# Retention, mixture of experts and a cosine layer on one core: the first unit's tiles joined by two engines, one transposed tile moved a slot

## The reference

```python
ret = scale * (q @ k.T) * Dmat            # gamma ** (i - j), lower triangle, 4 x 8 heads of 576 x 64
x = (ret @ v)                             # as 2304 rows of 512
noisy = x @ w_gate + log1p(exp(x @ w_noise)) * noise
top2 = two largest of the 8 experts; top2_w = softmax of the two
x = sum over the two: top2_w * (relu(x @ w1[e]) @ w2[e])      # 512 -> 1024 -> 512
h = x @ w_in                              # 512 -> 2048
out = (h * cos(h)) @ w_out                # 2048 -> 512
```

## Time and profile before

| what | value |
| --- | --- |
| median of 3 runs | 964.06 us (963.14 to 966.89) |
| profiled execution, its own time | 964.38 us |
| its span, first to last instruction | 962.5 us |
| TensorE busy | 936.7 us (97%) |
| VectorE, ScalarE busy | 560.2 us (58%), 534.7 us (56%) |
| mean granted TensorE clock | 0.987 |

### The profile page before, as it was taken

How to read it: one execution, slowest core, us unless ns; L and a number is a source line. 1 busy time by engine, 2 the same in 40 slices (tenths; PEclk the granted TensorE clock), 3 DMA queues, 4 the chain that set the end, 5 groups by cost and what they waited for, 6 DMA issues and landing times.

```text
span 962.5 us, 16768 instructions
## 1 busy us (share of the span) xinstructions
PE 936.7 (97%) x5984; PEld 834.6 (87%) x5984; DVE 560.2 (58%) x1118; ACT 534.7 (56%) x969; POOL 95.9 (10%) x93
## 2 busy tenths in 40 slices
PE   8999859999999999999999998999999999999998
PEld 8988858888888889898989888888988888888897
DVE  4788635465655555533331244567777777776665
ACT  2556537554655556453532256566757765766555
POOL 2276500000000000000000222001100100000000
PEclk9999879999999999999999999999999999999999
DMA  9999465779999999985427357877666755656561
GB/s 361 330 327 283 176 163 197 204 236 302 314 309 321 324 307 296 259 257 156 103 73 263 98 196 264 295 286 255 235 250 237 264 213 228 239 210 238 216 236 55
DMA packets 113113, 230.44 MB, mean 239 GB/s; under 512 B 47384, under 2 KB 71640, under 8 KB 104856
## 3 DMA queue, kind: packets, MB, share of 16 engines
q1 hardware_dynamic: 107288, 210.73, 65.6%
q0 software_dynamic: 5760, 18.88, 5.5%
HBM read 157.65 MB, written 61.70 MB: 228 GB/s over the span
## 4 chain that ended last, share of the span: by engine, by line
PE 76%; ACT 7%; DVE 7%; issue 4%; DMA 2%; POOL 1%; SPq 1%; DVEq 0%; POOLq 0%; ACTq 0%
PE ps L1708 17%; PE ps L1690 16%; PE ps L1877 13%; PE ps L1863 11%; PE ps L1791 3%; PE ps L1803 2%; PE ps L1614 2%; PE ps L1637 2%; ACT angle L984 2%; PE ps L1726 2%; PE ps L1629 2%; PE ps L1662 2%; DVE angle L1473 1%; ACT angle L982 1%; PE ps L1738 1%
## 5 line engine op out<-in xcount | busy, mean ns | idle before, releaser
L1877 PE MATMUL ps<-w_sb,g_hi 128*128 128x512 f32 x576 | 180.4, 394 | 0.1
L1690 PE MATMUL ps<-xs,w_hi 128*128 (+1 forms) x784 | 173.3, 303 | 0.8 <-DVE hs_lo L1297 0.8
L1690 PEld LDWEIGHTS ps<-xs,w_hi 128*128 128x128 f32 x784 | 131.2, 188 | 4.2 <-DVE hs_lo L1297 1.2
L1303 DVE TENSOR_TENSOR w_lo<-raw,w_hi 128x1024 fp32r<-128x1024 f32 x48 | 58.8, 1225 | 124.1 <-ACT w_hi L823 124.0
L1863 PE MATMUL ps<-x_odd,w_sb 128*128 128x320 f32 x672 | 117.7, 310 | 2.2 <-DVE h_sb L1458 1.2
L1863 PEld LDWEIGHTS ps<-x_odd,w_sb 128*128 128x128 f32 x672 | 106.2, 188 | 14.5 <-DVE h_sb L1458 2.5
L1690 PE MATMUL ps<-xs,w_lo 128*128 (+1 forms) x392 | 118.8, 303 | 0.0
L823 ACT ACTIVATE w_hi<-raw 128x1024 fp32r<-128x1024 f32 x48 | 50.9, 1060 | 118.0 <-PE ps L1708 113.1
L1877 PE MATMUL ps<-w_sb,g_lo 128*128 128x512 f32 x288 | 112.5, 391 | 0.0
L1877 PEld LDWEIGHTS ps<-w_sb,g_hi 128*128 128x128 f32 x576 | 101.0, 188 | 9.8 <-issue 0.3
L1708 PE MATMUL ps<-w_hi,hs_lo 128*128 128x512 f32 (+1 forms) x245 | 96.8, 395 | 0.0
(11 more groups left out here) (195 smaller groups left out, 1624.8 us busy)
## 6 DMA issues: line engine op xcount, KB each, us to landing
w_sb<-w_pairs SPq DMA_DIRECT2D x24, 1792.0 KB, 7.9
w_sb<-w_pairs SPq DMA_DIRECT2D x40, 1024.0 KB, 9.6
raw<-weights SPq DMA_DIRECT2D x64, 512.0 KB, 4.9
w_pairs<-stage SPq DMA_DIRECT2D x24, 1024.0 KB, 7.1
qk<-qk SPq DMA_DIRECT2D x18, 512.0 KB, 7.2
kv<-kv SPq DMA_DIRECT2D x18, 512.0 KB, 5.9
y_slots<-zeros_sb SPq DMA_DIRECT2D x33, 256.0 KB
raw_pair<-pairs SPq DMA_DIRECT2D x8, 1024.0 KB, 9.2
```

The costliest lines, as they stand in the source:

```text
L1303: tt(w_lo[:, at], raw[:, f % 2, :], w_hi[:, at].bitcast(F32), ALU.subtract).then_inc(split_done, 1)
L1690: last_one = nc.tensor.matmul(ps[5 + half][:, 0:HALF], w[:, at:at + P], xs[:, bass.ds(g % 2, 1), a, k, half * HALF:(half + 1) * HALF].rear ...
L1877: last_one = nc.tensor.matmul(ps[j][:, :], a[:, slot % 2, part, j * C:(j + 1) * C], w2_sb[slot % 3][:, hl, part * DM:(part + 1) * DM], sta ...
```

## The change

Unit 0's tiles are joined by two engines: ScalarE copies the lower plane (join in its stream), VectorE the upper (its own join, with a semaphore merged_dve). The tiles 2 to 4 get a buffer each, in raw_pair[1], in place of the one x_plain. On ScalarE the order in step 18 becomes: both joins, high part of tile 0, x_sb copy of tile 16, high part of tile 1. On VectorE the joins of tiles 0 and 1 stand ahead of second_choice and behind sum_picks. place_results goes behind the first h_low_first of part 1. From unit 1 on the joins stay on ScalarE. In block 0 of the last layer the third tile goes through one slot later on all engines.

```diff
--- before.py
+++ after.py
@@ -281,6 +281,7 @@
         passed, passed_sp = sem("passed"), sem("passed_sp")
         gath_in = [sem(f"gath_in{i}") for i in range(TPU)]
         merged, xs_hi_done, xs_done = sem("merged"), sem("xs_hi_done"), sem("xs_done")
+        merged_dve = sem("merged_dve")
         h_done, relu_done, hs_done = sem("h_done"), sem("relu_done"), sem("hs_done")
         p2_done, y_ready = sem("p2_done"), sem("y_ready")
         y_act, y_dve = sem("y_act"), sem("y_dve")
@@ -432,7 +433,19 @@
 
             if isinstance(g, int) and g == 0 and j < FRONT[0]:
                 return planes[FRONT[0] + j][:, :, :].rearrange("p a s -> p (a s)").bitcast(F32)
+            if isinstance(g, int) and g == 0:
+                return raw_pair[1][:, (j - FRONT[0]) * DM:(j - FRONT[0] + 1) * DM]
             return x_plain[:, :]
+
+        def half_of(g, j, h):
+
+            n = KD_TILES * ROWS[j]
+            return (x_raw(g, j)[:, 0:n].bitcast(U16).rearrange("p (k s h) -> p h k s", k=KD_TILES, h=2)[:, h, :, :],
+                    planes[j][:, h * KD_TILES:(h + 1) * KD_TILES, 0:ROWS[j]])
+
+        def joined(g, j):
+
+            return j + 1 if isinstance(g, int) and g == 0 else 2 * (TPU * g + j + 1) - TPU
 
         def steps_before(g):
 
@@ -562,14 +575,18 @@
             for j in range(FRONT[0], TPU):
                 load_rows(j, 0)
             for j in range(FRONT[0]):
-                sp.wait_ge(merged, 2 * (j + 1))
+                sp.wait_ge(merged, j + 1)
+                sp.wait_ge(merged_dve, j + 1)
                 load_rows(j, 1)
             for f in range(2):
                 load_chunk(RING + f, FE + f)
             for j in range(FRONT[0], TPU):
-                sp.wait_ge(merged, 2 * (j + 1))
+                sp.wait_ge(merged, j + 1)
+                sp.wait_ge(merged_dve, j + 1)
                 load_rows(j, 1)
             def load_pair(i):
+                if i == 1:
+                    sp.wait_ge(xs_done, TPU)
                 if i >= 2:
                     sp.wait_ge(pair_lo, 3 * (i - 1))
                 sp.dma_start(raw_pair[i % 2][:, :], pairs[i]).then_inc(pair_in[i % 2], 16)
@@ -592,14 +609,14 @@
                 e_next = nc.sync.value_load(meta[0:1, bass.ds(g + 1, 1)], min_val=0, max_val=E - 1)
                 v_next = nc.sync.value_load(meta[0:1, bass.ds(g + META_V + 1, 1)], min_val=0, max_val=NV - 1)
                 for j in range(2):
-                    sp.wait_ge(merged, 2 * (TPU * g + j + 1))
+                    sp.wait_ge(merged, joined(g, j))
                     sp.sem_inc(passed_sp, 1)
                     load_rows(j, v_next)
                 for j in range(TPU):
                     store_rows(g - 1, j)
                 for f in range(FE):
                     if 2 <= f < TPU:
-                        sp.wait_ge(merged, 2 * (TPU * g + f + 1))
+                        sp.wait_ge(merged, joined(g, f))
                         sp.sem_inc(passed_sp, 1)
                         load_rows(f, v_next)
                     load_ring(g, f, e_next)
@@ -768,19 +785,25 @@
                 if k < NG - 1:
                     nc.scalar.activation(sin_ready[:, :], tab("half_pi"), ACT.Exp)
 
+            def join(g, j):
+                act.wait_ge(gath_in[j], 16 * g + 16)
+                first = isinstance(g, int) and g == 0
+                if isinstance(g, int) and g == 1 and j == 0:
+                    act.wait_ge(y_pos_done, 1)
+                if not first:
+                    act.wait_ge(xs_done, TPU * g + j)
+                for h in range(1 if first else 2):
+                    to, half = half_of(g, j, h)
+                    nc.scalar.activation(to, half, ACT.Copy).then_inc(merged, 1)
+
             def x_high(g, j):
-                act.wait_ge(gath_in[j], 16 * g + 16)
-                if not isinstance(g, int) or g > 0 or j > FRONT[0]:
-                    act.wait_ge(xs_done, TPU * g + j)
-                n = KD_TILES * ROWS[j]
-                for h in range(2):
-                    nc.scalar.activation(
-                        x_raw(g, j)[:, 0:n].bitcast(U16).rearrange("p (k s h) -> p h k s", k=KD_TILES, h=2)[:, h, :, :],
-                        planes[j][:, h * KD_TILES:(h + 1) * KD_TILES, 0:ROWS[j]], ACT.Copy).then_inc(merged, 1)
-                act.wait_ge(merged, 2 * (TPU * g + j + 1))
+                act.wait_ge(merged, joined(g, j))
+                if isinstance(g, int) and g == 0:
+                    act.wait_ge(merged_dve, j + 1)
                 nc.scalar.activation(
                     xs[:, bass.ds(g % 2, 1), 0, :, rows_of(j)].rearrange("p a k s -> p (a k) s"),
-                    x_raw(g, j)[:, 0:n].rearrange("p (k s) -> p k s", k=KD_TILES), ACT.Copy).then_inc(xs_hi_done, 1)
+                    x_raw(g, j)[:, 0:KD_TILES * ROWS[j]].rearrange("p (k s) -> p k s", k=KD_TILES), ACT.Copy
+                    ).then_inc(xs_hi_done, 1)
 
             def step(s):
                 if s in SOFT_AT:
@@ -793,8 +816,9 @@
                     nc.scalar.activation(xT[t % 2][:, :, :], ps[O_BANK[t % 2]][:, :].rearrange("p (k c) -> p k c", k=KD_TILES),
                                          ACT.Copy).then_inc(xT_done, 1)
                 if t == NT - 1:
-                    for j in range(FRONT[0]):
-                        x_high(0, j)
+                    join(0, 0)
+                    join(0, 1)
+                    x_high(0, 0)
                 t = s - 2
                 if t == NT - 1:
                     softplus(NG - 1)
@@ -803,6 +827,8 @@
                     nc.scalar.activation(x_sb[t][:, :].bitcast(U16).rearrange("c (h d) -> c h d", h=2),
                                          ps[5][0:C, :].bitcast(U16).rearrange("c (d h) -> c h d", h=2), ACT.Copy
                                          ).then_inc(x_done, 1)
+                if t == NT - 2:
+                    x_high(0, 1)
                 if s in SPLIT_AT:
                     split_high(SPLIT_AT[s], w_hi, SPLIT_AT[s] * CHUNK)
 
@@ -853,12 +879,14 @@
                     act.wait_ge(g_ready, 1)
                     nc.scalar.activation(gate2[:, 0:NT], g_a[:, :], ACT.Exp).then_inc(g_done_exp, 1)
             for j in range(FRONT[0], TPU):
+                join(0, j)
                 x_high(0, j)
             for f in range(FE):
                 relu_first(f, 1)
                 if f > 0:
                     ring_high(f - 1)
                     if f <= TPU:
+                        join(1, f - 1)
                         x_high(1, f - 1)
             relu(FE, 0)
             y_rows(0)
@@ -886,6 +914,7 @@
                         y_rows(g)
                     w_high(g, f)
                     if f < TPU:
+                        join(g + 1, f)
                         x_high(g + 1, f)
                     if isinstance(g, int) and g <= PREP_UNITS:
                         pair_high(2 * (g - 1) + f // 4, f % 4)
@@ -1001,9 +1030,10 @@
                 first = FIRST_TILE[b + 1]
                 if b == 0:
                     if p == 2:
-                        for j in range(3):
+                        for j in range(2):
                             copy_raw(first + j)
                     if p == 3:
+                        copy_raw(first + 2)
                         prepare(first + 3)
                         prepare(first + 4)
                         x2_high(1, 0)
@@ -1044,6 +1074,7 @@
                 cosine(slot, 1)
                 if slot == 1:
                     prepare(FIRST_TILE[1] + 1)
+                if slot == 2:
                     prepare(FIRST_TILE[1] + 2)
             for slot in range(FP, SLOTS + 1):
                 b, p = slot // FP, slot % FP
@@ -1180,6 +1211,11 @@
                     nc.vector.tensor_tensor(ret[t % 3][rows, half, :, :], scores[rows, :, :],
                                             decay[rows, half, :, :], ALU.mult).then_inc(ret_done, 1)
 
+            def join(j):
+                dve.wait_ge(gath_in[j], 16)
+                to, half = half_of(0, j, 1)
+                nc.vector.tensor_copy(to, half).then_inc(merged_dve, 1)
+
             def carry(t):
                 c = t % CB
                 dve.wait_ge(u_done, updates(t) + 1)
@@ -1211,9 +1247,13 @@
                     carry(s - 1)
                 if s < NT and s % CB < CB - 1:
                     decay_k(s)
+                if s == NT:
+                    join(0)
                 if s in SECOND_AT:
                     second_choice(SECOND_AT[s])
                     sum_picks(SECOND_AT[s])
+                if s == NT:
+                    join(1)
                 if s in PLACE_AT:
                     place_rows(PLACE_AT[s])
                 if s in FIRST_AT:
@@ -1337,12 +1377,13 @@
                     list_units()
                 if f == 6:
                     gates()
-                if f == 7:
-                    place_results()
             for j in range(FRONT[0], TPU):
+                join(j)
                 x_low(0, j)
             for f in range(FE):
```

(8 more changed lines are left out.)

## The result

| | before | changed kernel |
| --- | --- | --- |
| median | 964.06 us (963.09 to 966.89, 5 runs) | 958.1 us (956.68 to 959.6, 5 runs) |
| ratio, 95% interval | | 0.9934 [0.9914, 0.9955] |
| profiled execution, its own time | 964.38 us | 958.10 us |
| its span | 962.5 us | 956.3 us |
| mean granted TensorE clock | 0.987 | 0.993 |

A forecast was written before the change was run, and what follows sets the result against it. TensorE bounds the kernel, working 936.7 of 962.5 us, so gains lie where it stands or runs at lower clock. 1.2 + 2.2 + 4.2 = 7.6 off 964.38 gives 956.8, median 956.5 us; range 953.5 to 960.8.

The forecast's parts named there:

- Front: Up to the experts' first product: joins shared by ScalarE and VectorE start it near 100.9 instead of 102.09, 1.2 us less.
- Late tiles: Unit 0's tiles 2 to 4: joins side by side in own buffers shorten the chain from 8.1 to 5.9, 2.2 us less.
- place_results and the clock: Part 1 and after restarts: moving place_results costs zero; both low-clock costs kept, a 3 us longer stretch costing 1.5 us.
- zero, nothing is moved past another transfer: SP's queue: waits come at the same points, met earlier, and load_pair(1) waits for late tiles long done; zero.
- a sign of being wrong: Unit 1: an unforeseen wait at the h_low behind place_results or at the ring loads would make the prediction wrong; no size.
- Block 0: Last layer, third tile one slot later: 2.7 us of standing and the lower clock behind it go, 4.2 us less.
- It waits for nothing: Slot 3 of block 0: third tile ready after 5.1 us, TensorE at its transposes after 6.3, 1.2 us to spare.
- the wait comes back: Block 0, slot 3 or 4: third tile's combine or the weights come late, 4.2 us falls away, 960.7; chance 0.11.
- The front's rival: VectorE's first copy, blocked by up to 0.96 us beside a scatter, delays second_choice; 0.2 of the term left, 957.5; chance 0.10.
- Slow copies with every other element: VectorE's five chain copies: from 2.2 us a copy the gain is gone, at 3.2 it ends at 969; chance 0.03.
- The late tiles don't land too slowly: Unit 0: late tiles land one by one and joins wait for them, the 2.2 falls to about zero, 958.7; chance 0.04.
- The clock's rival: Both restarts get the long low-clock stretch, or block 0's idle cost no clock in the typical run: 959; chance 0.08.

The follow-up runs named there:

- one_buffer: Changed kernel with both engines joining, but one x_plain for all late tiles and place_results back in its old place; 960.1 us, ratio 0.9946.
- place_back: Changed kernel with place_results back in its old place ahead of the late tiles; 958.75 us, ratio 0.9942.
- ring_first: Changed kernel with SP's first ring load of unit 1 issued ahead of the five stores of unit 0's rows; 957.49 us, ratio 0.992.
- prep_later: Changed kernel with scaling and combining of block 1's fifth tile in slot 3 placed behind x2_high and x2_low; 959.01 us, ratio 0.992.
- prep_turn: Changed kernel with block 1's fifth tile scaled behind the second half's turn of slot 3 and combined behind its reduce; 956.94 us, ratio 0.9912.
- tile: Kernel before with only block 0 changed, its third tile one slot later, unit 0 as before; 965.0 us, ratio 0.9981.
- unit0: Changed kernel with only the part on unit 0, block 0's third tile back in its old slots; 961.34 us, ratio 0.9949.

## Why the prediction came out as it did

The forecast was right in kind, and 1.6 us too far. That it came so near is in part luck: in the table above, the terms that turned out larger than forecast (front, late tiles, clock, block 0 up to slot 4) have 1.4 us in its favour, and those that it put at nothing 2.7 against it.

*Front (1.2 forecast, 1.66 measured).* The mechanism held: the low part of tile 1 sets the first product, behind ScalarE's row. The price of the VectorE copy, 0.45 in place of 0.68, isn't what the size was off by, since both copies are done before ScalarE's high parts want them. The sum added up whole durations on ScalarE: from the start of the joins to the end of the second high part 3.74 us (96.36 to 100.1). It measured 3.29 (96.64 to 99.93), because each instruction that waits for nothing begins some 0.1 us before the one ahead has ended. Those are the 0.45. The kernels with the new front all show 4.55 to 4.57 us from the last xT copy to the first product, also those in which TensorE waited 0.4 to 1.1 us for the x_sb copy. The exception is one_buffer with 5.18, where both engines begin their joins of tile 1 only at 99.39.

*Late tiles (2.2 forecast, 2.56 measured).* From the first join to the end of the last low part the sum had 5.9 us, and it measured 5.55. The two VectorE copies on this chain gave 0.17 of the difference, the low parts 0.23 and the high parts 0.06 (again each begins before the one ahead has ended), and ScalarE's first join took 0.11 more. The Trainium skill (VectorE: DVE Perf Modes, on the 2x mode with both ports) would have given 2.9 by its copy of 0.33 us. The measurement lies between: the copy takes 0.45 us for 512 elements and 0.39 for 416. I estimate from these two that 0.32 of the 0.45 goes with the length, and some 0.13 us is there whatever the length, near the smallest operations of the earlier trace rows (0.18). The same page remarks beside its table that the fixed part of a single operation was measured at about 150 cycles; from that I would have estimated 0.42, and the runs agree with it better. The three buffers or the second engine alone give some 70% of the gain (1.85 and 1.74 of 2.56), as the runs with one of the two show.

*place_results and the clock (0).* The first is confirmed by place_back. As for the clock, the stretch at 1.2 GHz behind the first product lasts to 104.5 (3.8 us, before 3.3) and the one behind the late tiles to 138.6 (5.4 us, before 6.2). The first costs under 0.1 us and the second gives 0.4, inside the 1.5 that I left open.

*SP, "zero, nothing is moved past another transfer".* **This step failed**, by 0.7 us in the profile and by 0.7 and 0.4 in the two repeats (in the other kernels that leave unit 1 alone, 0.02 to 1.04). Nothing was moved in SP's queue. The five stores begin at 172.25, 3.96 us earlier than before (176.21), as much as TensorE is ahead. But their issues take 3.70 us in place of 3.16, and from the load behind them to ScalarE's split of its weights it is 5.0 us in place of 4.8, so the split comes only 3.17 us earlier. ring_first shows that this queue bounds unit 1, as it did before the change. Why the stores and the load take longer now stays open. The prediction named a wait in unit 1 at the ring loads as a sign of being wrong, and didn't price it.

*Block 0 (4.2 forecast).* The gain up to slot 4 is right: 4.4 us, the standing of 2.7 and the clock. "It waits for nothing" is right too, in slot 3. **What failed is that the term ends there.** The prediction looked at the third tile's combine and the weights of slot 4, and put at nothing what comes next in ScalarE's queue in slot 3: the scaling of the fifth tile. Its gather goes out 3.4 us earlier, but takes 8.4 us in place of 3.8 and lands later than before. It holds ScalarE for 1.2 us, that delays the chain of ScalarE and VectorE in the slots 5 to 7, and TensorE pays 1.3 us there. It is near the rival "the wait comes back", but on another tile, a smaller wait, and without the clock. prep_later and prep_turn show the cause: with the wait the gain is 3.1, at 0.64 us of it 3.9, at none 4.8. The other traces fall in line: the longest wait, 2.29 us in one_buffer, leaves 2.0, and 1.96 us in tile leave 2.35.

*The rivals.* The front's rival (VectorE's first copy blocked beside a scatter) didn't come: where a copy began during a scatter it took 0.45 to 0.53 us, else 0.45. The Trainium skill (SBUF, Who interferes with whom) lets the one that comes second wait for the whole of the other. In these traces the price is 0 to 0.08 us, and not the 0.96 that I had bounded it by. Slow copies with every other element, the case that ends slower, are out by the same rows. The late tiles don't land too slowly either. The clock's rival didn't come in this profile, and its second half, that the idle of block 0 costs no clock, is what the trace of unit0 shows.

## What to carry to other kernels

When a stall is removed, the work behind it comes earlier, but what hangs on a transfer or on another queue may not come earlier by as much. So go through each in-order queue behind the place, and ask of every DMA that it waits for whether what sets it off moves along, and which other transfers now run beside it. Here one such wait came some 4 us behind the place and the other some 50. The two took back 2.0 us of 8.3, and moving one load and the handling of one tile brought more than both.

## What was not expected

- A two-byte copy to every other element (128x512) took 0.45 to 0.53 us on VectorE, and 0.74 to 0.78 on ScalarE, whether VectorE wrote the other half of the tile or not.
- Two of the profiled executions, tile and prep_turn, have a standstill of all engines near 94 us, in retention code that is the same in all kernels. VectorE in prep_turn:

```profile
96.19 0.42 DVE L1225 TENSOR_TENSOR state<-ps,attn_table 128x256 f32<-128x256 f32 x1 [3.00 <-remote]
```

  TensorE and ScalarE stand at the same time. It adds some 3 us to these two executions (961.16 for the profiled one of prep_turn, whose median is 956.94), so the parts of the change were measured between two events of one trace and not by the span. What causes it stays open.
- The time from the first product of the experts to the first join of a late tile varies from 25.9 us (tile) to 28.7 us (prep_later) between kernels whose code differs little there. What varies there stays open, and the spread is larger than most of the terms above.
